# A split-precision two-layer kernel: who makes the high part of g, how the cosine is made, and in which order a slot runs

## What is computed

```
out = einsum('hk,bskhg->bshg', softmax(weight), windows(x))      # 7 taps
h = out @ w_in;   g = h * cos(h);      x2 = g @ w_out            # layer A
h = relu(x2 @ w2_in);                  y  = (h * h) @ w2_out     # layer B
```

## Time and profile before

| | |
|---|---|
| median of 3 runs | 2639.35 us (2638.49 to 2639.89) |
| span of the profiled execution | 2636.2 us |
| PE busy | 2467.1 us (94%), 10880 matmuls |
| PEld busy | 2003.5 us (76%) |
| DVE busy | 2127.3 us (81%) |
| ACT busy | 1484.8 us (56%) |
| POOL busy | 682.4 us (26%) |
| mean granted TensorE clock | 0.985 of full speed |

### The profile page before, as it was taken

The page is one execution under the profiler, slowest core; times in us unless marked ns, Lnnn a source line. Parts: engine busy times, 40 slices in busy tenths (PEclk is TensorE's granted clock), DMA queues, the critical chain, the costliest instruction groups (busy, mean ns, idle before and its releaser), DMA issues. The chain is left out here.

```text
span 2636.2 us, 30240 instructions
## 1 busy us (share of the span) xinstructions
PE 2467.1 (94%) x10880; PEld 2003.5 (76%) x10880; DVE 2127.3 (81%) x2060; ACT 1484.8 (56%) x1549; POOL 682.4 (26%) x523
## 2 busy tenths in 40 slices
PE   5799999999999999999999999999999999999998
PEld 4577787777877777777777777778777778777787
DVE  7888888888888887888888888888888888888863
ACT  4455565655555555555555565555656556565554
POOL 2322222222222222222222222222222222222221
PEclk9899999999999999999999999999999999999999
DMA  3100000000000000000000000000000000000000
GB/s 101 36 1 13 13 6 12 12 6 12 12 6 12 6 12 12 12 6 12 6 12 12 6 12 12 6 12 12 6 12 6 12 12 6 12 12 6 6 7 13
DMA packets 39457, 32.89 MB, mean 12 GB/s; under 512 B 1676, under 2 KB 38668, under 8 KB 39180
## 3 DMA queue, kind: packets, MB, share of 16 engines
q1 hardware_dynamic: 39260, 32.61, 4.2%
q10 hardware_dynamic: 176, 0.00, 0.0%
HBM read 20.03 MB, written 12.58 MB: 12 GB/s over the span
## 5 line engine op out<-in xcount | busy, mean ns | idle before, releaser
L631 POOL TENSOR_SCALAR g_hi<-g 128x1024 fp32r<-128x1024 f32 x512 | 658.6, 1297 | 1920.6 <-DVE g L537 1612.2
L543 DVE TENSOR_TENSOR g_lo<-g,g_hi 128x1024 fp32r<-128x1024 f32 x512 | 744.4, 1459 | 167.7 <-POOL g_hi L631 162.0
L444 ACT ACTIVATE w<-w 128x1024 f32<-128x1024 f32 x256 | 271.5, 1061 | 751.2 <-DVE w L531 751.2
L537 DVE SCALAR_TENSOR_TENSOR g<-w,g 128x1024 f32<-128x1024 f32 x256 | 315.7, 1233 | 241.6 <-ACT w L446 239.0
L434 ACT ACTIVATE g<-h 128x1024 f32<-128x1024 f32 x256 | 261.3, 1021 | 268.1 <-PE h L322 268.1
L338 PE MATMUL y_A<-g_hi,dn_lo_A 128*128 128x512 f32 x512 | 222.0, 434 | 125.3 <-DVE g_lo L543 124.6
L531 DVE TENSOR_TENSOR w<-w,g 128x1024 f32<-128x1024 f32 x256 | 313.7, 1225 | 8.8
L436 ACT ACTIVATE g<-h 128x1024 f32<-128x1024 f32 x256 | 259.4, 1013 | 34.8 <-PE h L322 34.6
L438 ACT ACTIVATE g<-g 128x1024 f32<-128x1024 f32 x256 | 271.9, 1062 | 8.1
L446 ACT ACTIVATE w<-w 128x1024 f32<-128x1024 f32 x256 | 271.6, 1061 | 8.1
L570 DVE SCALAR_TENSOR_TENSOR conv_side<-xt_side,taps,conv_side 64x512 f32<-64x512 f32 x192 | 251.3, 1309 | 6.2
(11 more groups left out here) (90 smaller groups left out, 4669.3 us busy)
## 6 DMA issues: line engine op xcount, KB each, us to landing
rows_in<-x SPq DMA_DIRECT2D x32, 384.0 KB, 3.3
out<-late SPq DMA_DIRECT2D x32, 384.0 KB, 2.6
late<-w_out SPq DMA_DIRECT2D x2, 1536.0 KB, 10.2
g<-w_in SPq DMA_DIRECT2D x1, 1024.0 KB, 5.2
g<-w_in SPq DMA_DIRECT2D x2, 512.0 KB, 8.1
late<-w_in SPq DMA_DIRECT2D x2, 512.0 KB, 4.5
late<-w_in SPq DMA_DIRECT2D x4, 256.0 KB, 5.7
taps<-weight ACTq DMA_DIRECT2D x4, 0.7 KB
```

The lines of the kernel that those rows point to most:

```text
L444: act.activation(v, v, ACT.Sin, scale=math.pi).then_inc(sine, 1)
L537: dve.scalar_tensor_tensor(out=u, in0=v, scalar=1.0, in1=u, op0=ALU.subtract, op1=ALU.mult).then_inc(g_made, 1)
L543: dve.tensor_tensor(g_lo[:, r, :, :], g[:, r, :, :], g_hi[:, r, :, :].bitcast(F32), ALU.subtract).then_inc(lo_made[kind], 1)
L631: return pool.tensor_scalar(dst, src, 1.0, 0.0, ALU.mult, ALU.add)
```

## The change

The high part g_hi is made by ScalarE (`high_part`, an activation Copy), no longer by GpSimd, which keeps only the weight splits and makes them without g_hi between them. The cosine is one sine: VectorE adds a quarter turn in the rounding and takes off g in a two-step operation, and the sine gets scale and bias of a quarter turn from a column in SBUF; the square falls away, and the product with g becomes a plain one. The sign in layer A's down weights turns.

The order in a slot changes. ScalarE in slot s: `turned_cosine` of s-1, `read_h` of s, `high_part` of s-2. VectorE in slot s: `times_cosine` of s-1, `fraction` of s, taps, `low_part` of s-2. TensorE's program is the same.

```diff
-            def half_cosine(turn, p, back):
+            def turned_cosine(turn, p, back):
                 v = w[:, p % WB, :, :]
                 act.wait_ge(frac, turn.count("A", p, back))
-                act.activation(v, v, ACT.Sin, scale=math.pi).then_inc(sine, 1)
-                act.wait_ge(sine, turn.count("A", p, back))
-                act.activation(v, v, ACT.Square, scale=math.sqrt(2.0)).then_inc(sine_sq, 1)
+                act.activation(v, v, ACT.Sin, bias=quarter[:, 0:1], scale=-TURN).then_inc(cosine, 1)
+            def high_part(turn, e, kind, p, back):
+                r = turn.ring(e, back) % RING
+                before = Turn(turn.i - back, TILES, turn.i8 - NP * back)
+                freed = before.before(before.pairs, before.ring(e), RING)
+                if freed:
+                    act.wait_ge(used[freed[0]], freed[1])
+                act.wait_ge({"A": g_made, "B": relu_sq}[kind], turn.count(kind, p, back))
+                act.activation(g_hi[:, r, :, :], g[:, r, :, :], ACT.Copy).then_inc(hi_made[kind], 1)
...
             def body(turn):
                 for s, (kind, p) in enumerate(turn.slots()):
                     _, back, last, q = turn.earlier(s, 1)
-                    cosine = last == "A" and turn.runs("A", back)
-                    if cosine and not (kind == "A" and turn.runs("A")):
-                        half_cosine(turn, q, back)
+                    if last == "A" and turn.runs("A", back):
+                        turned_cosine(turn, q, back)
...
                     if turn.runs(kind):
                         read_h(turn, s, kind, p)
-                    if cosine and kind == "A" and turn.runs("A"):
-                        half_cosine(turn, q, back)
+                    e, back, made, q = turn.earlier(s, 2)
+                    if made in "AB" and turn.runs(made, back):
+                        high_part(turn, e, made, q, back)
...
             def fraction(turn, r, p):
-                dve.tensor_scalar(v, u, ROUND, ROUND, ALU.add, ALU.subtract).then_inc(whole, 1)
+                dve.tensor_scalar(v, u, 0.25, ROUND, ALU.add, ALU.add).then_inc(whole, 1)
                 dve.wait_ge(whole, turn.count("A", p))
-                dve.tensor_tensor(v, v, u, ALU.subtract).then_inc(frac, 1)
+                dve.scalar_tensor_tensor(out=v, in0=v, scalar=ROUND, in1=u, op0=ALU.subtract,
+                                         op1=ALU.subtract).then_inc(frac, 1)
             def times_cosine(turn, r, p, back):
-                dve.wait_ge(sine_sq, turn.count("A", p, back))
-                dve.scalar_tensor_tensor(out=u, in0=v, scalar=1.0, in1=u, op0=ALU.subtract,
-                                         op1=ALU.mult).then_inc(g_made, 1)
+                dve.wait_ge(cosine, turn.count("A", p, back))
+                dve.tensor_tensor(u, v, u, ALU.mult).then_inc(g_made, 1)
...
+                    if last == "A" and turn.runs("A", back):
+                        times_cosine(turn, r, q, back)
                     if kind == "A" and turn.runs("A"):
                         fraction(turn, turn.ring(s) % RING, p)
-                    if last == "A" and turn.runs("A", back):
-                        times_cosine(turn, r, q, back)
...
-                    if last in "AB" and turn.runs(last, back):
-                        low_part(turn, r, last, q, back)
+                    e, back, made, q = turn.earlier(s, 2)
+                    if made in "AB" and turn.runs(made, back):
+                        low_part(turn, turn.ring(e, back) % RING, made, q, back)
...
-            def body(turn):
-                for s, (kind, p) in enumerate(turn.slots()):
-                    e, back, last, q = turn.earlier(s, 1)
-                    if last in "AB" and turn.runs(last, back):
...
-                        round_hi(g_hi[:, r, :, :], g[:, r, :, :]).then_inc(hi_made[last], 1)
-                    if turn.peeled and turn.i == 0 and s in LATE_SLOTS:
-                        late_lo_part(1 + LATE_SLOTS.index(s))
-            turns(pool, body)
+            for n in range(1, 1 + len(LATE_SLOTS)):
+                late_lo_part(n)
```

More of the change, by code:

```diff
@@ L59 @@
 ROUND = 1.5 * 2.0 ** 23
+TURN = 13176794.0 * 2.0 ** -21
+QUARTER = 13176794.0 * 2.0 ** -23
 def at(t):
@@ L185, in tile_program @@
         tsum = sb("tsum", [P, 2])
+        quarter = sb("quarter", [P, 1])
         rows_loaded = sem("rows_loaded")
@@ L207, in tile_program @@
         taken = {k: sem(f"taken_{k}") for k in "ABXY"}
-        sine = sem("sine")
-        sine_sq = sem("sine_sq")
+        cosine = sem("cosine")
         relu_sq = sem("relu_sq")
@@ L225, in tile_program @@
         hi_made = {k: sem(f"hi_made_{k}") for k in "AB"}
-        pool_steps = sem("pool_steps")
         stage_in = g[:, :, :, :].rearrange("p r n t -> p (r n t)")
@@ L405, in late_hi @@
                 else:
-                    k, scale = ("A", -TWO_PI) if n == 0 else ("B", 1.0)
+                    k, scale = ("A", TWO_PI) if n == 0 else ("B", 1.0)
                     act.activation(dn_hi[k][:, :, :], stage_out[:, :, 0:P], ACT.Copy, scale=scale)\
@@ L492, in _ @@
             dve.memset(taps[0:P - SIDE, 1, :], 0.0).then_inc(zeroed, 1)
+            dve.memset(quarter[:, :], QUARTER).then_inc(zeroed, 1)
             dve.wait_ge(taps_loaded, 16 * TAP_DMAS)
-            dve.wait_ge(zeroed, 3)
+            dve.wait_ge(zeroed, 4)
             dve.tensor_reduce(tmax[:, :], taps[:, :, :], AX_X, ALU.max).then_inc(taps_step, 1)
@@ L517, in layer1_down_lo @@
                 dve.wait_ge(late_hi_made, 2)
-                dve.scalar_tensor_tensor(out=dn_lo["A"][:, :, :], in0=stage_out[:, :, 0:P], scalar=-TWO_PI,
+                dve.scalar_tensor_tensor(out=dn_lo["A"][:, :, :], in0=stage_out[:, :, 0:P], scalar=TWO_PI,
                                          in1=dn_hi["A"][:, :, :].bitcast(F32), op0=ALU.mult,
@@ L521, in layer1_down_lo @@
                 dve.scalar_tensor_tensor(out=dn_side["A"][:, :, SIDE:], in0=stage_out[:, :, P:D],
-                                         scalar=-TWO_PI, in1=dn_side["A"][:, :, 0:SIDE].bitcast(F32),
+                                         scalar=TWO_PI, in1=dn_side["A"][:, :, 0:SIDE].bitcast(F32),
                                          op0=ALU.mult, op1=ALU.subtract).then_inc(late_lo, 1)
@@ L626, in _ @@
         def _(pool):
-            def round_hi(dst, src):
-                pool.sem_inc(pool_steps, 1)
-                return pool.tensor_scalar(dst, src, 1.0, 0.0, ALU.mult, ALU.add)
             def late_lo_part(n):
```

## The result

The changed kernel takes 2803.28 us (median of 4 runs, 2799.21 to 2804.06) against 2639.11 us (4 runs) for the kernel before: a ratio of 1.0619, 95% interval 1.0604 to 1.0634. It is 6.2% slower; 2798 us had been forecast. Its profiled execution has a span of 2801.6 us, with a mean granted TensorE clock of 0.975 against 0.985 before.

The account below looks back on a forecast made before the run. TensorE's own work plus waits for late low parts was taken as the bound. Span 2636.2 + 108 + 2 + 9 + 22 - 7 + 25 = 2795, so 2798 us as median; range 2738 to 2848.

Parts of the forecast that it names:

- Rival 1: TensorE's low-part waits: freed engines win and all these waits go, 2494 us; chance 0.05.
- The two chains: From up product out to TensorE's start on the low part: 4.40 us in A slots, 4.55 in B.
- The waits: TensorE in a middle tile: five waits where a product is missing or slot 0's split delays, 7.84 us together.
- near-ties: Four ordinary slots per tile where the chain about equals TensorE's 4.53 us: 0.02 plus a 0.1 restart each, 0.5 together.
- The waits list: Profile's list of TensorE waits for the low part: about 280 us, of both layers.
- Turns 2 to 30: 29 middle tiles at 83.4 us, 3.7 more each than 79.67: 108 us added.
- Clock: Two waits over 2 us per tile instead of one, four in ten followed by a clock fall: +22 us.
- Rival 2: Every long wait drops TensorE's clock: 53 us more, 2850 us; chance 0.12.
- Start: Up to 99 us: later order costs some 2, GpSimd's free queue gives back about 9; -7 us.
- Turn 1 and turn 31: First full tile, which already had waits, +2 us; last one with A, without taps, +9.
- End: Last tile, only B: waits in slots with gaps, 20.5 less 2, plus four clock falls at 1.5; +25 us.
- What the freed engines bring: VectorE and ScalarE work saved was held off TensorE's path by itself, counting only where VectorE's lateness made the wait.

Follow-up runs that it names:

- engine_alone: Kernel before with only g_hi moved to ScalarE (of slot s-1), old cosine and old VectorE order: 2588.06 us, ratio 0.9811 to the kernel before.
- cosine_alone: Kernel before with only the new cosine (no square), g_hi on GpSimd and old order kept: 2468.22 us, ratio 0.9356 to the kernel before.
- order_with_gpsimd: Changed kernel with g_hi back on GpSimd (of slot s-1), new cosine and VectorE's new order kept: 2833.76 us, ratio 1.0749 to the kernel before.
- high_first: Changed kernel with only ScalarE's g_hi of s-2 moved to the head of its slot: 2703.73 us, ratio 1.0253 to the kernel before.
- one_slot_sooner: Changed kernel with high and low part of slot s-1 in place of s-2: 2486.99 us, ratio 0.9427 to the kernel before.
- both_first: Changed kernel with high and low part, still of s-2, both moved to the head of the slot: 2469.66 us, ratio 0.9361 to the kernel before.
- low_first: Changed kernel with only VectorE's low part of s-2 moved ahead of cosine product and fraction: 3253.38 us, ratio 1.2334 to the kernel before.
- cosine_and_engine: Kernel before with the new cosine and g_hi on ScalarE, both in the old order: 2489.09 us, ratio 0.9431 to the kernel before.
- old_cosine_new_order: Changed kernel with the old cosine (sine, then square) put back: 2903.00 us, ratio 1.1001 to the kernel before.

## Why the prediction held, point by point

- *What bounds it, and that the order decides*: right. Neither the engine nor the cosine makes the loss: engine_alone and cosine_alone both gain, and order_with_gpsimd loses with the engine left as it was. Rival 1, that the freed engines win, is out: the list of waits for low parts went from 125.9 us (124.6 + 1.3) to 244.4.
- *The two chains*: 4.40 (4.39 when its terms are added up) and 4.55 forecast, 4.41 and 4.58 measured.
- *The waits*: slot 8 2.28 forecast and 2.31 measured, slot 15 2.13 and 2.14. X (1.34), Y (1.03) and slot 1 (1.06) came out at 1.16, 0.84 and 0.77. Together that is 7.22 us against 7.84. The near-ties explain X and Y: the down product between the up product and X lost 0.18 itself (2.32 and 2.40 for 2.27 twice), and the chain runs meanwhile. In high_first, which has no near-ties, the same two waits are 1.34 and 1.04. My sum counted near-ties and waits as if they added. In slot 1 TensorE starts 5.32 us after the up product, not 5.6: `split_layer2` starts 0.14 us earlier and takes 2.46 us, not 2.59. The four near-ties are there, and cost 0.17 each (0.04 of wait and 0.13 of restart), 0.7 in place of 0.5. A tile without a fall of the clock is 83.10, 0.3 less than the 83.4 forecast.
- *The waits list*: about 280 us forecast, 244 found (137.0 + 107.4). The list counts idle time alone, which is 0.15 to 0.24 us less per wait than the start-to-start differences that I had summed, 28 us in 31 tiles; and the waits are the 0.6 us per tile smaller that were just named.
- *Turns 2 to 30*: 84.24 against 80.27 us per turn, 29 x 3.98 = 115, with the clock. Forecast 108 and most of 22: 13 too much.
- *Clock*: in turns 1 to 31 there are 24 falls (14 before); a tile with one takes 1.64 us more (84.74 against 83.10). 10 x 1.64 = 16, forecast 22. The count that I started from was off by one: of the 30 waits of slot 15 before, 13 are followed by slow steps, not 12. Rival 2, a fall at each long wait, didn't happen. The total is near the forecast by luck: I had given both long waits a fall in four of ten, 25 of 62. It was 22 of 62, but 19 of 31 behind slot 15's wait of 2.14 and 3 of 31 behind slot 8's longer one of 2.31. Why is open. A fall looks like this, the starts of the matmuls going from 0.24 to 0.37 us apart and then, in further rows, to 0.43:

```profile
1267.20 0.40 PE L342 MATMUL y_A<-g_hi,dn_hi_A 128*128 128x512 f32 x1
1267.44 0.58 PE L343 MATMUL y_A<-g_lo,dn_side_A 128*128 128x512 f32 x1
1267.81 0.63 PE L344 MATMUL y_A<-g_lo,dn_hi_A 128*128 128x512 f32 x1
```

The Trainium skill ("TensorE: Matmul & The Clock Gate", Part 1: The HAM clock gate) has the gate judge windows that run freely. Equal waits with and without a fall agree with that; the difference between slots 8 and 15 is not explained by it.

- *Start*: the step that failed. -7 was forecast, as +2 for the later order and -9 for the free queue; the first up product of turn 1 comes at 100.62 us against 99.45, +1.2. One_slot_sooner has the same engines and cosine without the later order, and has it at 91.60: -7.9, so the gain was about right. The term that was mis-sized is the order's, 9.0 us (100.62 - 91.60) where I took 2. Both_first, two slots late but behind nothing, has it at 100.45, so here it is the distance and not the place in the queue. The weight splits also still stretch VectorE (3.4 us for a low part of 1.2), as forecast.
- *Turn 1 and turn 31*: +4.1 and +14.3, forecast +2 and +9 without clock. Turn 31 has two falls (none before), turn 1 two as before; without them turn 31 is +11.
- *End*: +30.5, forecast +25. The pattern is as worked out, 4.55 us each in the slots named:

```profile
2751.57 0.50 PE L340 MATMUL y_B<-g_hi,dn_lo_B 128*128 128x512 f32 x1 [4.41 <-DVE g_lo L554]
```

  with five falls of the clock, 1.2 to 2.5 us each and 8.9 together, where I had four at 1.5.
- The measured parts sum to 1.2 + 4.1 + 115.3 + 14.3 + 30.5 = 165.4 = 2801.6 - 2636.2. The forecast of 2798 is 5 us off. That close it is luck: the start came out 8 us over, turns 2 to 30 with their clock 13 under, turn 31 and the end 5 over each, and these cancel. The waits and the chains behind the 3.7 us per tile are no luck.
- *What the freed engines bring*: I took the new cosine at nothing and the contention at nothing. In the new order the contention is small (with g_hi on GpSimd it is 30 us more), but the cosine isn't (with the old one it is 100 us more). In the old order they were worth 50 and 170 us, since there the closed loop, not a single chain, was the limit. The prediction didn't need it, since it asked only about the changed kernel. Cosine_alone, engine_alone, low_first and high_first, where a loop or a second queue counts, missed their expected times; cosine_and_engine, both_first and one_slot_sooner, where nothing of the kind is left in the middle, met theirs (one_slot_sooner to 12 us).

## What to carry to other kernels

When a step is moved in an in-order queue, look at what the instruction ahead of it waits for, and add up the chain from that event to the consumer; then compare it with the bounding engine's time between the two, at each place in the schedule where that time is short (a slot with a product missing), not in the mean. Then close every path through the queues into a loop and compare its round with the bound's round: four rounds of 36.9 us against TensorE's 32.8 went with 170 us here, and a round of 11.1 us against 9.1 with a loss of 614, while the busy shares showed idle engines everywhere. A change made of three parts can hold gains and a loss: here 6% up with all three, 6% down without the third. And the gains need not add: with the new cosine in place, moving g_hi gave nothing more and cost 21 us.

## What the runs showed of the hardware

- Two-source operations of VectorE and operations of GpSimd stretch each other. Without GpSimd the side tap takes 752 ns instead of 1309, the split of x_side_A 688 instead of 1389, the low part 1232 instead of 1459. The Trainium skill ("GPSIMD Engine Reference", 1. Specifications) says that GpSimd shares its SBUF interfaces with VectorE and contends with two-input instructions; the traces agree, with these sizes. Beside GpSimd's weight splits of 2.5 to 3.4 us it is more: 3.4 us for a low part (at 47.41 us of the changed kernel), and 2.86 for the fraction's first step (at 66.54; 0.69 otherwise), although that has one source.
- The sine with a bias column takes 1151 ns instead of 1061. I had left this between 0 and 0.2 us. The Trainium skill ("ScalarE: Activation LUTs", What ACT_TABLE_LOAD costs) gives some 93 ns for a pointer operand; the 90 ns here agree.
- The length of TensorE's wait doesn't by itself say whether the granted clock falls behind it. Waits of 2.03 to 2.08 us were followed by a fall in 13 of 30 tiles (before), of 2.14 in 19 of 31 and of 2.31 in 3 of 31 (changed), of 2.13 in 3 of 29 (high_first), of 2.35 in 18 of 29 (engine_alone), of 2.7 in 24 of 30 (old_cosine_new_order). These are start-to-start times.
